# Attention, routing and experts on one core: products with V over 128 keys at once, V held twice, routing in eight parts, early scatters unpaced

## The reference

```python
def _attn_ref(q, k, v):                       # (4, 8, 576, 64) each
    scores = scale * np.matmul(q, k.transpose(0, 1, 3, 2))
    rel = pos[:, None] - pos[None, :]
    scores = np.where((rel >= 0) & (rel < 64), scores, -1e9)
    attn = softmax(scores)                    # with 1e-9 added to the sum
    return np.matmul(attn, v)

def _moe_ref(x, w_gate, w_noise, noise, w1, w2):   # x (2304, 512), 8 experts, F 1024
    noisy = x @ w_gate + np.log1p(np.exp(x @ w_noise)) * noise
    # the two largest of each token's eight, weighted by a softmax over the two
    # out[token] += weight * (relu(x @ w1[e]) @ w2[e])

def _moe2_ref(x, w_in, w_out):                # d_ff 2048
    h = x @ w_in
    return (h * np.clip(h + 3.0, 0.0, 6.0) / 6.0) @ w_out
```

## Time and profile before

| | |
|---|---|
| median of 3 runs | 1141.75 us (1141.51 to 1143.86) |
| profiled execution | 1144.95 us, span of its instructions 1143.1 us |
| mean granted TensorE clock | 0.964 |
| PE, PEld busy | 92%, 78% |
| DVE, ACT, POOL busy | 35%, 25%, 34% |
| PE matmuls and weight loads | 7856, 7857 |

### The profile page before, as it was taken

How to read it: one execution, slowest core, us unless ns; L and a number is a source line. 1 busy time by engine, 2 the same in 40 slices (tenths; PEclk the granted TensorE clock), 3 DMA queues, 4 the chain that set the end, 5 groups by cost and what they waited for, 6 DMA issues and landing times. The chain is left out here.

```text
span 1143.1 us, 22070 instructions
## 1 busy us (share of the span) xinstructions
PE 1046.7 (92%) x7856; PEld 887.7 (78%) x7857; DVE 404.4 (35%) x832; ACT 280.4 (25%) x582; POOL 392.5 (34%) x247
## 2 busy tenths in 40 slices
PE   5888843999999999999999995899999999999998
PEld 4666633888888888888888774798998989989897
DVE  2455554212222121222212213454444535444433
ACT  3566631122122122212212213112111111111111
POOL 1221264557455472909183651720010101000000
PEclk9998966999999999999999998799999999999999
DMA  9774524633333251414243232231010110100000
GB/s 202 147 155 127 193 95 162 243 128 114 115 101 128 78 161 43 159 64 156 73 128 111 94 127 67 102 90 47 19 38 28 37 46 20 35 28 1 28 1 28
DMA packets 80229, 106.27 MB, mean 93 GB/s; under 512 B 26928, under 2 KB 45360, under 8 KB 80176
## 3 DMA queue, kind: packets, MB, share of 16 engines
q1 hardware_dynamic: 61408, 64.34, 19.7%
q10 hardware_dynamic: 13008, 22.29, 6.0%
q0 software_dynamic: 5760, 18.88, 5.0%
HBM read 76.91 MB, written 28.57 MB: 92 GB/s over the span
## 5 line engine op out<-in xcount | busy, mean ns | idle before, releaser
L1309 PE MATMUL PS<-W,xs 128*128 (+1 forms) x960 | 236.7, 402 | 6.1 <-issue 4.3
L1343 PE MATMUL PS<-W,hs 128*128 x960 | 234.4, 400 | 1.4 <-DVE hs L1012 1.4
L550 POOL TENSOR_TENSOR W<-stage,ones_f 128x1024 fp32r<-128x1024 f32 x74 | 141.1, 1906 | 270.8 <-PE PS L1343 184.4
L1390 PE MATMUL PS<-x2s,W 128*128 128x384 f32 x1152 | 220.2, 339 | 1.5 <-DVE x2s L1064 1.5
L1406 PE MATMUL PS<-W,gs 128*128 128x512 f32 x864 | 215.7, 394 | 4.1 <-issue 2.4
L1309 PEld LDWEIGHTS PS<-W,xs 128*128 128x128 f32 x960 | 179.5, 190 | 48.3 <-issue 7.6
L1390 PEld LDWEIGHTS PS<-x2s,W 128*128 128x128 f32 x1152 | 205.1, 189 | 8.8 <-issue 1.9
L1343 PEld LDWEIGHTS PS<-W,hs 128*128 128x128 f32 x960 | 177.7, 188 | 41.7 <-issue 1.6
L1406 PEld LDWEIGHTS PS<-W,gs 128*128 128x128 f32 x864 | 160.3, 188 | 35.5 <-issue 6.3
L552 POOL TENSOR_TENSOR W<-stage,W 128x1024 fp32r<-128x1024 f32 x74 | 177.6, 2401 | 5.8
L772 ACT ACTIVATE gs<-g 128x384 fp32r<-128x384 f32 x96 | 50.6, 527 | 312.3 <-DVE g L1073 307.8
(11 more groups left out here) (148 smaller groups left out, 672.5 us busy)
## 6 DMA issues: line engine op xcount, KB each, us to landing
stage<-in_moe_w_dram SPq DMA_DIRECT2D x64, 512.0 KB, 3.9
x_in<-x_sorted ACTq DMA_DIRECT2D x43, 256.0 KB
y_sorted<-y_sb ACTq DMA_DIRECT2D x40, 256.0 KB, 2.1
vD<-in_v_dram SPq DMA_DIRECT2D x32, 144.0 KB, 5.5
out_dram<-o_sb SPq DMA_DIRECT2D x18, 256.0 KB, 2.2
stage<-in_moe_w_in_dram SPq DMA_DIRECT2D x8, 512.0 KB, 4.0
stage<-in_moe_w_out_dram SPq DMA_DIRECT2D x8, 512.0 KB, 5.0
q_raw<-in_q_dram SPq DMA_DIRECT2D x5, 512.0 KB, 4.6
```

Of the source, the lines that this page charges most:

```text
L550: nc.gpsimd.tensor_tensor(hi, raw, ones_f[:].broadcast_to([P, CH]), ALU.mult).then_inc(w_half, 1)
L1309: last = nc.tensor.matmul(HP_[:, n, :], xs[:, a, kd, :], W[:, bass.ds(par, 1), 0, b, at:at + BANK].rearrange("p o n -> p (o n)"), start=fi ...
L1343: last = nc.tensor.matmul(YP, hs[:, a, c * P:(c + 1) * P], W[:, bass.ds(par, 1), 1, b, c * DM:(c + 1) * DM].rearrange("p o n -> p (o n)"), ...
L1390: last = nc.tensor.matmul(H2P[:, c % 2, :], W[:, 0, kd // 2, b, at:at + P], x2s[:, par, a, kd, :], start=first, stop=(kd == KD - 1 and (a, ...
```

## The change

- `times_v` takes 128 keys at once: 16 products in a tile, one for each head and half, on half of PE's array (128 rows by 64 columns).
- V is held in two arrangements, a ring of six tiles each. In arrangement 1 the even block of a tile lies on partitions 0 to 63, its odd block on 64 to 127 (for s = 1). Arrangement 0, for s = 0, has the odd block of the tile before on 64 to 127. It is filled by two DMAs for each tile from SBUF to SBUF (`second_v`). V is loaded by two DMAs for each tile.
- Keys, masks and probabilities follow the same order of blocks, so each product of the scores is one matmul.
- SP's list becomes one regular loop: q and k three chunks ahead, `second_v` one tile ahead, V three tiles ahead, weight chunks at `FIRST_AT`.
- Routing has eight parts. `route` is placed ahead of `normalise` for parts 0, 1, 2, 4, 5 and 6, and behind `move_ga` for 3 and 7; the ranks come an iteration later (7 after the lot's last tile, before 6).
- The scatters of lots 0 and 1 no longer wait for PE. POOL splits chunks 4 and 5 between the scatters of lots 0 and 1, and chunks 6 and 7 between those of lots 1 and 2; ACT and DVE split none of them.
- ACT loads one table set that holds both exponential and logarithm ahead of its list.

```diff
-    RT = 3 * CT
+    RB = 6
+    RV = 6
+    FIRST_AT = (1, 3, 5, 7, 13, 14, 15, 16)
-    BY_ACT = 2
-    vD = over("vD", [P, 2, KB, HP, VW])
+    vD = over("vD", [P, 2, RV, H, VW])
...
+            def load_v(t):
+                if t >= RV:
+                    sp.wait_ge(out_full, t - RV + 2)
+                for s in range(2):
+                    b, i = half(t, s)
+                    sp.dma_start(vD[WIN * s:WIN * (s + 1), 1, t % RV, :, 0:D],
+                                 v[b, :, i * WIN:(i + 1) * WIN, :].rearrange("h p d -> p h d")).then_inc(v_full[t % RV], 16)
+            def second_v(t):
+                sp.wait_ge(v_full[t % RV], v_there(t))
+                if t == 0:
+                    sp.wait_ge(v_ones, 1)
+                if t >= RV - 1:
+                    sp.wait_ge(out_full, t - RV + 2)
+                sp.dma_start(vD[0:WIN, 0, t % RV], vD[0:WIN, 1, t % RV]).then_inc(v_second[t % RV], 16)
+                if t + 1 < TILES:
+                    sp.dma_start(vD[WIN:P, 0, (t + 1) % RV], vD[WIN:P, 1, t % RV]).then_inc(v_second[(t + 1) % RV], 16)
...
+            load_v(2)
+            second_v(0)
+            for T in range(TILES):
+                iteration(T)
+                if T % 2 == 0 and T // 2 + 3 < CHUNKS:
+                    load_qk(T // 2 + 3, both)
+                if T + 1 < TILES:
+                    second_v(T + 1)
+                if T + 3 < TILES:
+                    load_v(T + 3)
+                if T == 4:
+                    sp.dma_start(noise_sb[:], noise.rearrange("(t p) e -> p t e", p=P)).then_inc(s_small, 16)
+                if T in FIRST_AT:
+                    load_first(FIRST_AT.index(T))
...
             scatter(0)
+            pool.wait_ge(ld_full, ITEMS)
+            for c in range(QCH, QCH + 2):
+                pool.wait_ge(stage_full[c % STAGES], 32)
+                split(0, c, c, c + 1)
             scatter(1)
+            for c in range(QCH + 2, SCH):
+                pool.wait_ge(stage_full[c % STAGES], 32)
+                split(0, c, c, c + 1)
             scatter(2)
...
+            nc.scalar.preload_act_table_set("natural_log_exp_and_others")
...
-                for n in due(T, 6):
-                    route(n, 4)
+                for after, parts in ((7, (5, 6)), (3, (0,)), (4, (1,)), (5, (2,)), (6, (4,))):
+                    for n in due(T, after):
+                        for part in parts:
+                            route(n, part)
                 if 1 <= T <= TILES:
                     normalise(T - 1)
-                for n in due(T, 3):
-                    route(n, 0)
-                for n in due(T, 4):
-                    route(n, 1)
-                for n in due(T, 5):
-                    route(n, 2)
-                    route(n, 3)
-                for n in due(T, 6):
-                    route(n, 5)
                 if 2 <= T <= TILES + 1:
                     move_ga(T - 2)
+                for after, part in ((5, 3), (7, 7)):
+                    for n in due(T, after):
+                        route(n, part)
...
-                for hp in range(HP):
-                    for n in range(2):
-                        for s in range(2):
-                            b, i = half(T, s)
-                            if i == 0 and n == 0:
-                                continue
-                            at = (2 * (hp % 2) + n) * P + s * WIN
-                            for x in range(2):
-                                part = slice(x * D, (x + 1) * D)
-                                last = nc.tensor.matmul(OUT[s * WIN:(s + 1) * WIN, x, hp, :],
-                                                        pT[part, T % 2, hp // 2, at:at + WIN],
-                                                        vD[part, b % 2, i - 1 + n, hp, 0:D + 1],
-                                                        start=(n == 0 or i == 0), stop=(n == 1), skip_group_check=True)
+                for h in range(H):
+                    for s in range(2):
+                        keys = slice(s * WIN, (s + 1) * WIN) if half(T, s)[1] == 0 else slice(0, P)
+                        at = (h % HP) * P + s * WIN
+                        last = nc.tensor.matmul(OUT[s * WIN:(s + 1) * WIN, h % 2, h // 2, :],
+                                                pT[keys, T % 2, h // HP, at:at + WIN], vD[keys, s, T % RV, h, 0:D + 1],
+                                                start=True, stop=True, skip_group_check=True)
```

More of the change, by code:

```diff
@@ L223, in attention_moe_ffn @@
         raw_full = [sem(f"raw_full{i}") for i in range(RAWS)]
-        v_full = [sem(f"v_full{i}") for i in range(B)]
+        v_full = [sem(f"v_full{i}") for i in range(RV)]
+        v_second = [sem(f"v_second{i}") for i in range(RV)]
         ld_full = sem("ld_full")
@@ L637, in move_first @@
                 act.wait_ge(ld_full, n + 1)
-                nc.scalar.copy(ring(n, 0), turned(n, 0)).then_inc(ld_act, 1)
+                nc.scalar.copy(ring(n, 0), moved_from(n, 0)).then_inc(ld_act, 1)
             def exps(T):
@@ L720, in _ @@
             load_x(0, first=True)
-            for c in range(SCH - BY_ACT, SCH):
-                at = slice((c % QCH) * CH, (c % QCH + 1) * CH)
-                act.wait_ge(stage_full[c % STAGES], 32)
-                nc.scalar.copy(W[:, 0, 1, 0, at], stage[:, c % STAGES, :]).then_inc(w_hi_act, 1)
             x_hi(0)
@@ L947, in _ @@
             nc.vector.tensor_scalar(first_pad[:], step_f[:, 2, 0:1], 1.0, None, ALU.add).then_inc(early_ready, 1)
-            for part in range(6):
+            for part in range(8):
                 route(NB - 1, part)
@@ L1151, in scores, with product @@
                                          start=True, stop=False, skip_group_check=True)
-                def product(s, x, hp, n, blocks):
+                def product(s, x, hp):
                     rows = slice(x * D, (x + 1) * D)
-                    qt = (2 * T + s) * WIN % RT
-                    kt = (2 * T + s - 1 + n) * WIN % RT
-                    at = hp * P + n * WIN
-                    return nc.tensor.matmul(SC[s * WIN:(s + 1) * WIN, T % 2, x, at:at + blocks * WIN],
-                                            qkT[rows, hp, 0, qt:qt + WIN], qkT[rows, hp, 1, kt:kt + blocks * WIN],
-                                            start=False, stop=True, skip_group_check=True)
+                    own, e = T % RB, (T if s else T - 1) % RB
+                    blocks = qkT[rows, hp, 1].rearrange("p a i w -> p (a i) w")
+                    if half(T, s)[1] == 0:
+                        at, keys = hp * P + s * WIN, qkT[rows, hp, 1, s, own, :]
+                        dst = SC[s * WIN:(s + 1) * WIN, T % 2, x, at:at + WIN]
+                    else:
+                        keys = blocks[:, own:RB + e + 1:RB + e - own, :]
+                        dst = SC[s * WIN:(s + 1) * WIN, T % 2, x, hp * P:(hp + 1) * P].rearrange("p (a w) -> p a w", w=WIN)
+                    return nc.tensor.matmul(dst, qkT[rows, hp, 0, s, own, :], keys, start=False, stop=True,
+                                            skip_group_check=True)
                 for hp in range(HP):
@@ L1178, in transpose_p @@
                     pe.wait_ge(pt_moved, 2 * T + g)
-                for h in range(2):
-                    for n in range(2):
-                        at = (2 * h + n) * P
-                        last = nc.tensor.transpose(PT[:, at:at + P],
-                                                   probs[:, T % 2, 2 * g + h, n].rearrange("p x w -> p (x w)"), ident[:])
+                for h in range(HP):
+                    last = nc.tensor.transpose(PT[:, h * P:(h + 1) * P], probs[:, T % 2, HP * g + h, :], ident[:])
                 last.then_inc(pt_full, 1)
@@ L1266, in _ @@
                     transpose_p(T, 0)
-                for n in due(T, 6):
+                for n in due(T, 7):
                     rank(n, T)
```

146 lines of the change are left out of this document (42 added, 104 removed).

## The result

The changed kernel takes 1160.76 us (median of 4 runs, 1157.28 to 1163.05), the one before 1142.33 us in the same rounds: a ratio of 1.0157, 95% interval 1.0127 to 1.0187. It is slower by 18.4 us; 1120 us was forecast. The profiled execution took 1159.59 us (span 1157.9).

A forecast was written before the change was run, and what follows sets the result against it. The bound was the handover, where PE waits for block 0's load behind POOL's queue. The start of T = 16 (-15.4 us) and POOL's chain (-6.4) took 21.8 off 1141.75: 1120 us, range 1106 to 1135.

The forecast's parts named there:

- What bounds it: Handover to the experts: time moves as much as block 0's load, which waits for POOL's queue; 182.2 to 160.4 us.
- The products with V: `times_v` in the loop: 32 matmuls in two halves take 1.09 us as before, no gain or loss in the array.
- The rival: `times_v`: halves do not run side by side, 1140 us at 2.2 us each or 1185 at 4.7; chance 0.08.
- the short tile: Loop, T = 2 to 15: shares 3.5 us of remaining excess with scatters beside PE and a lock of DVE.
- The unpaced scatters: POOL's chain: 10 scatters of lot 1 and 8 of lot 2 at 1.27 us each, 12.7 and 10.2 us.
- a lasting stall not seen here: Anywhere in the kernel: the part of the 0.07 chance of a slower result not due to the halves, 0.03.
- The loop without them: T = 2 to 15: 13 clean iterations of 5.69 us plus 12 us of excess, 10.6 us less than before.
- Routing in pieces: DVE's routing around the gate copies: 6.5 us of excess off in the loop, and T = 15 4.8 us shorter.
- V's copies: 35 new DMAs of 139 KB in the loop: 0.34 us each, 12 us together, hidden behind PE.
- ACT's table loads: ACT: fewer table loads left at nothing, since in the loop ACT waits for PE anyway.
- The lock: T = 14: POOL's splits of chunks 4 and 5 slow DVE's part 2 of lot 1; +4 us, between 0 and +6.
- POOL's chain behind T = 16: From the start of T = 16 to block 0's load: 39.8 us in place of 46.2, -6.4 us.

The follow-up runs named there:

- e1: The changed kernel with all 128 keys in every product with V, zero probabilities covering the missing block: 1148.54 us, ratio to before 1.0048.
- e2: The changed kernel with the scatters of lots 0 and 1 waiting for PE's progress again, two an iteration: 1145.78 us, ratio to before 1.0015.
- e4: The kernel before with only the waits of lots 0 and 1's scatters for PE taken out: 1151.75 us, ratio to before 1.0079.
- e3: The changed kernel with both 128 keys in every product with V and paced early scatters: 1134.39 us, ratio to before 0.9917.
- e7: The kernel before with routing in the smaller pieces and nothing else: 1139.52 us, ratio to before 0.9968.
- e14: e3 with V copied out once more to unused memory, 36 more DMAs of 139 KB: 1139.01 us, ratio to before 0.9978.
- e13: e3 with four early scatters an iteration and chunks 4 to 7 split by ACT and DVE after the first load: 1124.86 us, ratio to before 0.9845.
- e5: e3 with chunks 6 and 7 split by ACT and DVE after the first load instead of by POOL: 1127.25 us, ratio to before 0.9846.
- e6: The changed kernel with all eight 64-key products first in the four tiles where a sequence starts: 1150.50 us, ratio to before 1.0062.
- e9: e3 with ten plain 256 KB copies of x tiles issued by POOL before its paced scatters: 1138.49 us, ratio to before 0.9950.

## Why the prediction was wrong

**What bounds it: right.** The time moved with the load of block 0: 13.5 us there and 1.3 behind it make the 14.8 us between the spans of the two profiled executions (1159.59 and 1144.95 us, 14.6 apart). The medians are 18.4 apart, for the profiled one of before lay 2.6 us above its median of these rounds, that of after 1.2 below.

**The products with V: the step that failed.** "16 a half ... 1.09 us once more" was applied to 18 tiles; it holds in 14 (1.15 us at full clock). The rival asked whether the two halves run side by side, and they do; what it costs to alternate two shapes stood in no term but "the short tile", a part of 3.5 us. The four mixed tiles were in the diff: `keys` is a half for one `s` and everything for the other, inside the loop over `h`. They cost 12.2 us (e1), by about 3 us in each and by the slow clock behind three of them.

**The unpaced scatters: the second step that failed.** "8 x 1.27", "10 scatters x 1.27 = 12.7" were counted on POOL, and nothing on PE but a share of 3.5 us. Removing the waits cost 15.0 us (e2; in the kernel before 8.6, e4), because scatters in an unbroken row hold up PE. The 0.03 for "a lasting stall not seen here" is all that the prediction gave to such a thing. No row of before could show its price: there every unbroken row stood where PE had nothing to do.

**The loop without them: right.** e3 takes 113.06 - 27.54 = 85.5 us from T = 2 to T = 15; the forecast was 86.0 (13 clean iterations and 12). The two starts in its timeline:

```profile
27.54 0.41 PE L1136 MATMUL PS<-masks,ident_b 64*64 64x512 bf16 x4
...
113.06 0.41 PE L1136 MATMUL PS<-masks,ident_b 64*64 64x512 bf16 x4
```

T = 16 starts at 118.97, forecast 120.6, in part by luck: the 4 us of lock in that sum did not come there, while T = 2 starts 1.9 us late and T = 15 takes 5.9 us for 5.05. At the start the wait for k is gone, but T = 2 comes at 27.5 for 25.6: PE waits 1.86 us for ACT's exponentials instead.

**Routing in pieces: right in kind, too large.** In e3 PE's waits for the gate copy at T = 10 and 11 are gone; alone the pieces are worth 3.8 us (e7) where 11 were assumed. Part of what they free is waited for elsewhere, on the logits' copy (1.1 to 5.6 us).

**V's copies: right to leave PE's waits out**, with a price of up to 5 us by e14 in place of none. **ACT's table loads**, left at nothing, fall from nine (11.6 us of ACT) to one (1.3 us); no run takes them apart from the rest.

**The lock: right in the changed kernel.** POOL's splits of chunks 4 and 5 (132.80 to 141.40) stand in T = 14 and 15 beside part 2 of lot 1. All four of its operations read two tensors in SBUF (the prediction counted three), and all four are caught; in e3, with no split beside them, they take 0.2 us each. Timeline of DVE in the kernel after:

```profile
133.36 1.39 DVE L858 TENSOR_TENSOR noisy<-lnp,place 128x40 f32<-128x40 f32 x1
134.78 2.39 DVE L859 SCALAR_TENSOR_TENSOR nsp<-logits,noisy 128x40 f32<-128x40 f32 x1
137.21 1.82 DVE L860 TENSOR_TENSOR expz<-nsp,noise_sb 128x40 f32<-128x40 f32 x1
139.06 2.40 DVE L861 TENSOR_TENSOR noisy<-expz,logits 128x40 f32<-128x40 f32 x1
```

That is 8.0 us, the forecast's worst case being 8.7. T = 15 takes 148.68 - 139.48 = 9.2 us, where the forecast had 5.05 and 4 of lock. 2.4 us of it are PE's waits for DVE and part is the slow clock behind the mixed tile, so the sum is met, and the split between the two is not known. So of the 28.1 us that are missing at T = 16, 27.9 lie ahead of T = 15: T = 2 starts 2.7 us late (28.29), and T = 2 to 15 take 111.2 us for 86.0.

**POOL's chain behind T = 16: too small.** In e3 the chain takes 169.32 - 118.97 = 50.4 us for 39.8, though the last part (scatters of lot 2 to the load) is 13.4 as forecast. The rows of e3 (timeline, DVE and POOL):

```profile
122.32 2.36 POOL L553 TENSOR_TENSOR W<-stage,W 128x1024 fp32r<-128x1024 f32 x1
122.47 2.27 DVE L889 TENSOR_TENSOR nsp<-hot,place 128x40 f32<-128x40 f32 x1
...
126.85 2.12 DVE L891 COPY slot_x<-slot_f 128x10 f32<-128x10 f32 x1
...
129.33 1.01 POOL L569 DMA_INDIRECT x_sorted<-x_cur,slot_cur  x1 [0.38 <-DVE slot_cur L892]
```

The slots of lot 1 are made beside the splits of chunks 4 and 5. Three of the six operations from 122.47 on take 1.6 to 2.3 us, each until POOL's operation ends, and the slots come 10.4 us into T = 16 for 4.0. In e3 the splits start later, at 120.34, and so the lock stands here, at 6.4 us, and not in T = 14; PE waits 5.6 us for the gate copy behind it. Pacing stretches lot 1 to 17.8 us for 12.7. Of the 14 us between e3 and the forecast 8.9 are the load, 3.2 the offset of the profiled execution of before, which the forecast took off, and 2.0 lie behind the load (962.9 us for 960.9), their cause not found. With no split on POOL at all (e13) the load is at 162.57, still 2.2 us later than the prediction had it with four. There T = 16 starts at 125.71, 5.1 us late, after the crawl under four scatters an iteration, and the chain of 36.9 us is 5.8 longer than the forecast's 39.8 less 8.7. So what the forecast missed in the chain is what pacing and a late routing add to it, not the time of the splits themselves.

The 8.7 us that chunks 6 and 7 take POOL were in the sum; undoing that part alone is worth 7.1 us by the medians (e5).

## What to carry to other kernels

Count changes of the matmul's shape, not only matmuls: where two shapes must be mixed, issue all of one shape and then all of the other (e6), or pad the smaller with zeros (e1). A wait that paces one engine's queue may be what another engine lives by; before taking it out, look in the trace for a place where the unpaced row stood beside the other engine's work, and if there is none, the price is unknown, not zero. Work put on the engine whose queue ends last can be paid twice, when it also locks the engine that feeds that queue.

## What the hardware showed

Alternating matmuls of 64*64 and 128*64 cost 0.20 us a change at full clock, of which 0.14 goes with the change (e6) and the rest with the halves no longer side by side. Within such a row of fifteen changes the granted clock falls from 1.00 to 0.50 in three of four places (1.12 us for 0.66 in the transposes behind), with e6's one change in none. Ten indirect scatters at 1.27 us one behind another hold PE at one to five matmuls each 0.7 to 1.6 us, whether their rows have 2048 bytes or 64, and DVE goes on 7.0 us after PE's result is there (105.3 to 112.31); four in a row, behind ten plain copies, already do it (e9). With pauses of 1 to 3 us between them (e3) the iterations take 5.9 to 7.0 us. A DVE operation that takes 0.2 to 0.5 us elsewhere takes up to 2.4 us beside one of POOL's splits, also one on a single row:

```profile
146.63 2.44 DVE L931 TENSOR_SCALAR step_f<-iota_s,base_e 1x43 f32<-1x43 f32 x1
147.13 1.91 POOL L551 TENSOR_TENSOR W<-stage,ones_f 128x1024 fp32r<-128x1024 f32 x1
```
